# The attention head of a fused kernel: scores a beat ahead, values last in a beat, slopes in their beats, another load order

## What is computed

```python
# attention: B, H, S, D = 4, 8, 576, 64; window = 128
scores = q @ k.T / sqrt(D)
bias = slopes[h] * -abs(i - j)                  # slopes[h] = 2 ** -(h + 1)
scores = where(0 <= i - j < window, scores + bias, -1e9)
attn = softmax(scores)                          # sum + 1e-9
x = (attn @ v)                                  # 2304 tokens x 512
# MLP: w_in 512 x 2048, w_out 2048 x 512
x = (s * relu(x @ w_in) ** 2 + b) @ w_out
# mixture: 8 experts, two a token, w1 512 x 1024, w2 1024 x 512
logits = x @ w_gate + log1p(exp(x @ w_noise)) * noise
out = sum over the top two experts of weight * (relu(x @ w1[e]) @ w2[e])
```

## Time and profile before

| | |
|---|---|
| median of three executions | 1161.19 us (1160.66 to 1162.18) |
| profiled execution, own time | 1160.35 us |
| its span | 1158.5 us |
| TensorE busy | 1072.5 us, 93% |
| VectorE busy | 678.1 us, 59% |
| ScalarE busy | 476.7 us, 41% |
| mean granted clock | 0.974 |
| bytes moved | 146.90 MB, mean 127 GB/s |

### The profile page before, as it was taken

One profiled execution on the slowest core, in us unless ns is written; L12 is line 12 of the kernel. 1 busy time (PEld: TensorE's weight loads), 2 busy tenths in 40 slices (PEclk: granted clock), 3 DMA queues, 4 the chain that ended last, 5 costly groups with the idle time before them and its releaser, 6 DMA issues.

```text
span 1158.5 us, 20528 instructions
## 1 busy us (share of the span) xinstructions
PE 1072.5 (93%) x6751; PEld 963.5 (83%) x6752; DVE 678.1 (59%) x2006; ACT 476.7 (41%) x1036; POOL 137.8 (12%) x135
## 2 busy tenths in 40 slices
PE   4489799999999999999973999999999999999995
PEld 3478788888888888888963999999999999999994
DVE  5777666867766776754655636463644537454342
ACT  5656555555556555544531314231413314132111
POOL 0000000010020020010012121212111211212121
PEclk9799999999999999999995999999999999999998
DMA  6349922333342242132352515261522516233232
GB/s 214 91 150 349 365 92 83 109 132 97 101 137 83 83 159 80 46 110 84 117 182 92 183 36 168 75 202 56 175 75 94 198 66 205 94 130 110 68 107 73
DMA packets 80238, 146.90 MB, mean 127 GB/s; under 512 B 12924, under 2 KB 13564, under 8 KB 80176
## 3 DMA queue, kind: packets, MB, share of 16 engines
q1 hardware_dynamic: 70256, 125.36, 33.7%
q0 software_dynamic: 9920, 20.78, 5.2%
HBM read 111.14 MB, written 46.77 MB: 136 GB/s over the span
## 4 chain that ended last, share of the span: by engine, by line
PE 82%; DVE 6%; issue 4%; ACT 4%; SPq 2%; DMA 2%; POOL 0%; POOLq 0%; DVEq 0%; ACTq 0%
PE bank L1103 24%; PE bank L1104 23%; PE bank L1105 23%; PE bank L1084 3%; PE bank L1224 2%; PE bank L1071 2%; PE bank L1129 1%; PE bank L1050 1%; PE bank L1051 1%; ACT x_sc L519 1%; DVE x_sc L700 1%; SPq L351 1%; DMA stage_a<-in_w_second 1%; DVE x_sc L714 1%; ACT w_now_hi L558 1%
## 5 line engine op out<-in xcount | busy, mean ns | idle before, releaser
L658 ACT ACTIVATE g_hi<-bank 128x256 fp32r<-128x256 f32 x176 | 67.7, 384 | 348.4 <-PE bank L1105 329.9
L995 DVE SCALAR_TENSOR_TENSOR g_lo<-bank,g_hi 128x256 fp32r<-128x256 f32 x176 | 74.5, 423 | 183.5 <-ACT g_hi L658 183.4
L1103 PE MATMUL bank<-w_hi,g_hi 128*128 128x512 f32 x336 | 135.9, 404 | 0.0
L1104 PE MATMUL bank<-w_lo,g_hi 128*128 128x512 f32 x336 | 131.9, 392 | 0.0
L1105 PE MATMUL bank<-w_hi,g_lo 128*128 128x512 f32 x336 | 131.1, 390 | 0.0
L564 ACT ACTIVATE relu<-bank 128x384 f32<-128x384 f32 x96 | 47.1, 490 | 166.1 <-PE bank L1105 157.0
L1103 PE MATMUL bank<-xm_hi,w_hi 128*128 128x256 f32 x384 | 109.5, 285 | 1.5 <-DVE xm_lo L930 1.5
L1104 PE MATMUL bank<-xm_lo,w_hi 128*128 128x256 f32 x384 | 109.7, 286 | 0.0
L1105 PE MATMUL bank<-xm_hi,w_lo 128*128 128x256 f32 x384 | 109.6, 285 | 0.0
L462 POOL DMA_INDIRECT rows_scratch<-x,slot x36 | 38.9, 1081 | 556.5 <-DVE x L827 547.4
L742 DVE SCALAR_TENSOR_TENSOR relu<-relu,sb_scale 128x384 f32<-128x384 f32 x96 | 59.3, 617 | 65.2 <-ACT relu L564 63.3
(11 more groups left out here) (177 smaller groups left out, 2766.3 us busy)
## 6 DMA issues: line engine op xcount, KB each, us to landing
stage_a<-in_w_first SPq DMA_DIRECT2D x92, 256.0 KB
stage_a<-in_w_second SPq DMA_DIRECT2D x92, 256.0 KB
y_scratch<-x SPq DMA_DIRECT2D x41, 512.0 KB, 7.9
qk_raw<-in_qk SPq DMA_DIRECT2D x144, 128.0 KB, 2.7
rows<-rows_scratch SPq DMA_DIRECT2D x23, 516.0 KB
stage_b<-in_w_first SPq DMA_DIRECT2D x28, 256.0 KB
stage_b<-in_w_second SPq DMA_DIRECT2D x28, 256.0 KB
v_sb<-in_vp SPq DMA_DIRECT2D x18, 256.0 KB, 3.1
```

The source lines that it names most:

```text
L658: act.activation(g_hi[:, c % GR, 0:TOK2], h_bank[c % 2][:, 0:TOK2], ACT.Relu).then_inc(gh2_ready, 1)
L995: dve.scalar_tensor_tensor(out=g_lo[:, c % GR, 0:TOK2], in0=h_bank[c % 2][:, 0:TOK2], scalar=0.0, in1=g_hi[:, c % GR, 0:TOK2].bitcast(F32) ...
L1103: pe.matmul(psum, lh, rh, start=(first and n == 0), stop=False)
L1104: pe.matmul(psum, lh, rl, start=False, stop=False)
```

## The change

Unit scores are issued one beat ahead: TensorE issues scores 0, then in beat i scores i + 1, transposes i - 2, and at the end, in beats 6, 10 and 14, a block's values. `s_of` keeps three banks up to `LEAD` = 15. ScalarE and VectorE get a `head_beat` of their own: `x_of_block` and `rest_of_x` of blocks 0 and 1 stand one beat later (7 and 11), that of block 2 stays in beat 14, at its end. Ahead of the beats ScalarE makes splits and slopes of units 0 and 1 only; those of 2 and 3 stand in beats 0 and 1, and so does the split of unit (1,0). `seam_f` lies in `stage_a`, so `copy_t` no longer waits for the cast. The weight rounds 0 and 1, values of block 2 and the constants are loaded in beats 4, 5, 6 and 8; round 1 waits for the cast.

```diff
-        seam_f = pT[:, 1:3, :].rearrange("p u c -> p (u c)")[:, 0:5 * P]
+        seam_f = stage_a[:, 1, 0:5 * P]
-            return (s_bank, bank[0], bank[3])[i % 3] if i < FREE else s_bank
+            return (s_bank, bank[0], bank[3])[i % 3] if i < LEAD else s_bank
 # SyncE
+                load_v(0)
                 sp.dma_start(seam_f, a["seam"]).then_inc(seam_in, 16)
-                load_v(0)
                 load_v(1)
-                load_round(sp, 0)
-                load_round(sp, 1)
-                load_v(2)
-                for to, name in (...):
-                    sp.dma_start(to[:], a[name]).then_inc(const_in, 16)
                 for i in range(LEAD):
                     beat(i)
+                    if i == 4:
+                        load_round(sp, 0)
+                    if i == 5:
+                        sp.wait_ge(seam_cast, 1)
+                        load_round(sp, 1)
+                    if i == 6:
+                        load_v(2)
+                    if i == 8:
+                        for to, name in consts:
+                            sp.dma_start(to[:], a[name]).then_inc(const_in, 16)
 # ScalarE
                     if i < HP:
                         act.wait_ge(nbias_cast, H)
-                        act.wait_ge(seam_cast, 1)
+                def head_beat(i):
+                    exps(i)
+                    if i > WEIGH and (i - 1 - WEIGH) % HP == 0:
+                        x_of_block((i - 1 - WEIGH) // HP)
+                    if i >= TURN:
+                        copy_t(i - TURN)
+                    if i + 2 < HP:
+                        split(0, i + 2)
+                        slopes(i + 2)
+                    if i == 1:
+                        split(1, 0)
+                    if i >= 1:
+                        split(i // HP + 1, i % HP)
+                    if i == LEAD - 1:
+                        x_of_block((i - WEIGH) // HP)
-                for hp in range(HP):
+                for hp in range(2):
                     split(0, hp)
                     slopes(hp)
                 for i in range(LEAD):
-                    beat(i)
+                    head_beat(i)
 # VectorE
+                def head_beat(i):
+                    add_bias(i)
+                    if i >= 1:
+                        normalise(i - 1)
+                    if i > WEIGH and (i - 1 - WEIGH) % HP == 0:
+                        rest_of_x((i - 1 - WEIGH) // HP)
+                    if i + 2 < HP:
+                        rest_of_qk(0, i + 2)
+                    if i >= 1:
+                        rest_of_qk((i - 1) // HP + 1, (i - 1) % HP)
+                    if i == LEAD - 1:
+                        rest_of_x((i - WEIGH) // HP)
                 for i in range(LEAD):
-                    if i < UNITS:
-                        add_bias(i)
-                    if i == 0:
-                        rest_of_qk(0, 2)
-                        rest_of_qk(0, 3)
-                    after_scores(i)
+                    head_beat(i)
 # TensorE
-                    if i > FREE:
+                    if i > LEAD:
                         pe.wait_ge(biased, i)
-                    elif i == FREE:
-                        pe.wait_ge(biased, FREE - 2)
+                    elif i == LEAD:
+                        pe.wait_ge(biased, LEAD - 2)
                     elif i >= 3:
                         pe.wait_ge(biased, i - 2)
                         if t == 0 and c == 0:
-                            pe.wait_ge(biased, FREE)
+                            pe.wait_ge(biased, LEAD)
+                scores(0)
                 for i in range(LEAD):
-                    before_mlp(i)
+                    if i + 1 < LEAD:
+                        scores(i + 1)
                     after_mlp(i)
+                    if i >= WEIGH and (i - WEIGH) % HP == 0:
+                        weigh_values((i - WEIGH) // HP)
```

More of the change, by code:

```diff
@@ L364, in _ @@
                     load_raw(1, hp)
+                load_v(0)
                 sp.dma_start(seam_f, a["seam"]).then_inc(seam_in, 16)
-                load_v(0)
                 load_v(1)
-                load_round(sp, 0)
-                load_round(sp, 1)
-                load_v(2)
-                for to, name in ((sb_scale, "scale_bias"), (w_route, "w_route"), (noise, "noise"),
+                consts = ((sb_scale, "scale_bias"), (w_route, "w_route"), (noise, "noise"),
                                  (before_f, "before"), (iota_e, "iota_e"), (region, "region"),
                                  (iota_g, "iota_g"), (edge, "edge"), (token, "token"),
-                                 (row_no, "row_no")):
-                    sp.dma_start(to[:], a[name]).then_inc(const_in, 16)
+                                 (row_no, "row_no"))
                 def beat(i):
```

## The result

The changed kernel takes 1153.38 us (median of 6, 1151.85 to 1154.33), the one before 1160.93 beside it (median of 6). The ratio is 0.9938, with a 95% interval of 0.9925 to 0.9951: 5.7 to 8.7 us faster, where 1153.1 was forecast. The profiled execution is the slowest of the six: 1154.33 us, span 1152.5, against the 1152.3 and 1150.4 of the prediction. The two profiled executions differ by 6.0 us, which lies inside that interval too.

What follows compares the result with a forecast made beforehand. VectorE sets the head's beat, with 9.4 us of waits for scores. Beats sum to 19.6 us at bias 4 plus 36.7: first product at 56.3, all 8.1 us passed on, median 1153.1, range 1150.0 to 1156.8.

Steps and rivals of the forecast that it cites:

- What sets the beat: Head's loop: where nothing is late, VectorE sets the pace, with bias passes 2.51 us apart.
- three waits behind the weighing: VectorE's idle times before bias passes, for scores queued behind weigh_values: 9.4 us in all, expected to go.
- Slopes: Beats 0 and 1: slopes moved into the beats cost 1.7 us, bias 2 at 14.4 us instead of 12.70.
- Seam: Beat 3: GpSimd's cast and memset, from about 16.0 to 18.1 us, delay VectorE's normalising by 1.0 us.
- Load order: Loads of q and k, weights and constants: new order costed at nothing, with 2 us cover before beat 12.
- Beats 7 and 11: Block 0 and 1 x work moved here: VectorE waits 0.7 us for x_hi, 3.83 us per beat against 3.12.
- The step that finds no wait behind a weighing of up to 3.60 us: Beats 6, 10, 14: weighing last leaves the next scores in time, scores 12 ready at 41, wanted at 42.1.
- Or the weighing at the low level lasts longer, which is hidden: Alternative within the clock rival: weighing at the 1.2 GHz level takes longer but costs nothing.
- Beats 12 to 14: End of head: beats 12 and 13 stay 5.01 us each; beat 14 takes 4.15 instead of 3.25, costing 0.9.
- The sum: Head's beats added up: first product at 56.3 us instead of 64.44, 8.1 us earlier.
- Passed on: After the head: all 8.1 us reach the end, since the full transfer stretch moves along with its start.
- clock rival: At 73.6 to 77.2 us the 1.2 GHz stretch may not occur: gain 9.9, 1151.3 us; 12 in 100.

Runs made afterwards that it cites:

- experiment 1: Kernel before with only the new TensorE order; slopes, seam and loads as before: median 1153.65 us, ratio 0.9939.
- experiment 2: Changed kernel with slopes and splits of units 2 and 3 ahead of the beats again: median 1150.92 us, ratio 0.9912 to the kernel before.
- experiment 7: Kernel before with GpSimd's memset of x2 ahead of the wait for the seam: median 1162.08 us, ratio 0.9992.
- experiment 3: Changed kernel with GpSimd's memset of x2 ahead of the wait for the seam: median 1150.78 us, ratio 0.9912 to the kernel before.
- experiment 6: Changed kernel with the ten constants loaded ahead of the beats again: median 1157.24 us, ratio 0.9957 to the kernel before.
- Experiment 4: Changed kernel with pT as a ring of five units instead of four: median 1152.66 us, ratio 0.9926 to the kernel before.
- Experiment 5: Changed kernel with x_hi of block 2 first in beat 14, ahead of copy and split: median 1153.00 us, ratio 0.9918 to the kernel before.
- all four: Changed kernel with early slopes, memset before the seam's wait, five places in pT, block 2's x_hi first in beat 14: median 1149.62 us, ratio 0.9888.

## Why the prediction was right, point by point

**What sets the beat.** Right. Where nothing is late, bias passes are 2.51 us apart in every trace. The three waits behind the weighing are gone, and experiment 1 shows that this is nearly the whole gain.

**Slopes.** Right: bias passes 1 and 2 were forecast at 10.2 and 14.4 and came at 10.13 and 14.23; experiment 2 prices the part at 1.65, the sum had 1.7.

**Seam.** Right that the memset would stop VectorE, wrong in place, and low in size. It was forecast at 16 to 18 us in beat 3 and came at 19.36, in beat 4. SyncE's loads of block 1's q and k each wait for `qk_ready` of a unit of block 0, the last for unit 3, whose split the slopes now delay; the seam stands behind them. I costed the order of the queue and not its waits. It took 1.5 us (3.85 against 2.36), I had 1.0. The pass it stopped was the small addition, not the normalising. The 1.7 us of the earlier trace rows also were not what the memset cost the kernel before: ScalarE's wait for the cast held beat 3 up as well (3.70 us in experiment 1, where the memset stopped no pass; 2.99 in experiment 7, without the memset there; 2.11 in the changed kernel), and the wait for the load of unit (2,0) took up the rest. By the Trainium skill, "SBUF — State Buffer", "Who interferes with whom", whoever gets the shared port pair first keeps it for the whole instruction and the other stands still. The trace agrees so far as a one-tensor pass of 0.16 us took 1.64 and ended with the memset; experiment 3 shows which instruction held it, not through which port.

**Load order.** Costed at nothing; no load was late in beat 12 (the split of (4,0) didn't wait). What it gains was not in the sum either: experiment 6 puts the constants' place alone at 1.6 us, and beat 5 of experiment 1, with all loads in the old order, was 2.35 us longer than in the changed kernel.

**Beats 7 and 11.** Beat 7 was 3.97 against 3.83. Beat 11 is the term that was mis-sized: 5.36 against 3.83. The step that finds no wait behind a weighing of up to 3.60 us, since the scores behind it are in time, looked only at who waits for scores. It left out `act.wait_ge(pv_done, i // HP)` in `copy_t`: the weighing that moved behind the transposes also frees `pT` later. Experiment 4 shows it, and its wait follows the weighing's length: 1.42 us at 2.92, 1.63 at 3.19, 1.86 at 3.36, 2.15 to 2.18 at 3.65 to 3.68. The length itself follows the granted clock. Windows over block 1's weighing in the changed kernel, in experiment 1 and in experiment 2, and over two later weighings of 32 matmuls in the changed kernel:

```profile
36.61:39.97 3.36, 3.36 (x34) 3.19 (x33) 3.18 (x17) 1.18 (x5) 0.00 (x0) 0.57 0.31 63
...
37.65:40.57 2.92, 2.92 (x34) 2.75 (x33) 2.81 (x15) 1.19 (x5) 0.00 (x0) 0.66 0.32 93
...
35.47:39.14 3.67, 3.67 (x34) 3.34 (x33) 3.49 (x18) 1.19 (x5) 0.00 (x0) 0.52 0.31 63
...
105.47:107.44 1.97, 1.97 (x33) 1.80 (x33) 0.89 (x3) 0.42 (x1) 0.00 (x0) 1.00 1.05 379
139.39:143.07 3.68, 3.68 (x33) 3.35 (x33) 2.35 (x5) 1.37 (x2) 0.00 (x0) 0.50 0.58 165
```

So the 1.2 GHz level lay over most of this weighing, and the prediction's "Or the weighing at the low level lasts longer, which is hidden" was wrong too.

**Beats 12 to 14.** 5.01, 5.02 and 4.16 us against 5.01, 5.01 and 4.15. Experiment 5 shows the 0.9.

**The sum.** 56.3 forecast, 58.38 measured; of the 2.1, beat 11 is 1.5, beat 7 0.14, and 0.3 stand at bias pass 5: 0.5 more for the memset, less 0.2 for an earlier bias pass 2. The head gained 6.1 us where I had 8.1. The forecast of the median hit all the same, since the median fell by 1.5 more than the head; that part was luck within the runs' spread, not a step of mine.

**Passed on.** Right. Span less first product is 1094.1 us before and after, and 1094.9 with all four. The transfer stretch moved with the head. The clock rival did not happen: the 1.2 GHz stretch is there, 3.4 us long as before.

## What to carry to other kernels

When an operation is moved to the end of a step, list everybody who waits for it, not only those queued behind it: those who want its result, and those who want the buffer that it reads. Do the same for a load: its place in the queue counts for little if the loads in front wait for semaphores that the change itself makes late. A stall found in a profile has a price only while nothing else covers it; taking the same memset away gained nothing in one order and 0.7 us of the head in the next, where its beat had been 1.5 us longer for it.

## What the runs showed of the hardware that was not expected

- A VectorE addition of 128x2, 0.16 us elsewhere, took 1.64 us beside GpSimd's cast and 1.38 us memset; with the memset moved to the start (0.72 us into the span) it was short again. Beside the 0.72 us cast of 128x640 a VectorE subtraction of 128x256, 0.43 us elsewhere, took 0.95.
- The 32 small matmuls of one block's weighing took 1.97 us at a granted clock of 1.00 and 3.68 at 0.50. In the head block 1's took 2.90 to 3.68 in the ten traces, at a mean granted clock of 0.66 to 0.50; length times clock is 1.8 to 1.9 us in all of them. Why the level rose earlier in some than in others, with TensorE's order the same in eight of the ten, stays open.
- The part after the head varied between profiled executions (span less first product 1092.8 to 1096.6 us) though its order was the same in all; what sets that was not settled.
